# Eight first-layer products, one weight piece and one task's means moved earlier in the lead-in of a fused attention and two-mixture kernel

## The chip, the cores and the metric

The kernel runs on one core of one Trainium2 chip, as one program. The metric is the device time of that program in microseconds (us); the value given for a kernel is the median of its runs.

## What is computed

Three stages follow one another on N = 1536 rows of 512 values (batch 2, sequence 768, 8 heads of 64):

```python
# attention: a band of 15 keys either side, and one summary key per block of 32
k_sum = k.reshape(B, H, nb, block, D).max(axis=3)
v_sum = v.reshape(B, H, nb, block, D).mean(axis=3)
scores_l = scale * (q @ k^T), kept where |i - j| < 16
scores_s = scale * (q @ k_sum^T) + log(32)
x = softmax([scores_l, scores_s]) @ [v, v_sum]
# first mixture, 4 experts, all of them for every row
out += p[:, e:e + 1] * (np.maximum(x @ w1[e], 0.0) @ w2[e])
# second mixture, 8 experts: rows with x @ w_skip > 0 go to the expert of the
# largest logit, the result is added with that expert's probability
```

## The kernel before

**Tasks.** Attention is done in 16 tasks; task a covers one pair of heads and one half (384 rows) of a sequence. Tasks 0 to 3 (`LEAD = 4`) are the four head pairs of the first half, and make the 4 x 128 input columns of the first group of 384 rows of the first mixture. These four are done in the lead-in, before there is any mixture work; tasks 4 to 15 are interleaved with the mixture's first expert.

A task has two halves h (the heads of its pair). On TensorE: `transpose_keys`, `transpose_queries`, `qk(a)` (scores, L1772), `turn(a, h)` (transposes of the probabilities, L1786, after `norm(a, h)`), `pv(a)` (values, L1800). On VectorE: `keys(a)` (the block maxima), `mask(a, h)` (mask and row maximum, L1126), `norm(a, h)` (L1134, L1136, L1138), `low_o(a)` (L1144). On ScalarE: copies of keys and queries, `exps(a, h)` (L864), `evac_t(a, h)` (L870), `high_o(a)` (L875). GpSimd and SyncE issue transfers.

**Two parts for every number.** The mixture's products are made in a fast format. Each operand is split in a high part (rounded to that format) and a low part (the rest), and three products are summed: high by high, high by low, low by high. For the activations, `high_o` and `low_o` make `xt_hi` and `xt_lo`. For w1 of expert 0, GpSimd makes the high part (`high_w1`, a cast, L737) and VectorE the low part (`low_w1`, a subtraction, L1193), piece by piece: piece kc is rows 128 kc to 128 kc + 127 of w1, with all 1024 columns. An F block is 128 of those columns; there are 8. A product of F block f and piece kc is one matrix product of 128 x 128 by 128 x 384.

**Order of work.** It is written by hand for each engine, and semaphores join the engines. GpSimd, on its one queue, copies the block means of the values into the value tiles (`first_sums(a)`, two transfers, L732), loads the pieces of w1 (`first_w1(c)`, L723) and casts them. `first_sums(a)` for a of 2 or 3 waits for `pv(a - 2)`, since it fills the tile which that one read; `pv(a)` waits for it, for the values' windows (`load_windows`, from SyncE), for both `evac_t` of the task, and for `low_o(a - 1)`. `first_w1(1)` waits for the second block of means (`vsum_ok` of 2).

TensorE's lead-in ends with `lead(2)`, that is turn(2,0), qk(3), the queries of task 4, pv(1), turn(2,1), and then

```python
            turn(LEAD - 1, 0)
            pv(LEAD - 2)
            turn(LEAD - 1, 1)
            qk(LEAD)
            pv(LEAD - 1)
```

After that it runs `attend(4, ...)`: the queries of task 5, then `group_steps` for the first group (L1846, L1849, L1852 are F block 0, L1738 to L1740 the others), then turn(4,0), qk(5), turn(4,1). The first two F blocks come before turn(4,0).

VectorE's end of the lead-in is norm(2,1), mask(3,1), norm(3,0), low_o(1), norm(3,1), low_w1 of piece 0, low_o(2), low_w1 of pieces 1 and 2, low_o(3), low_w1 of piece 3, mask(4,0), mask(4,1), norm(4,0). `spare` puts transposes of the identity into some of TensorE's waits (L1889).

Of the kernel before, what the change touches and what calls it, by code (L numbers as in the profile page):

```python
# [15 lines left out]
P = 128  # L16


def sparse_attention_moe_moe(nc, q, k, v, dprobs, w1, w2, w_skip, w_gate, v1, v2, out):
# [102 lines left out]
    with ExitStack() as ctx:  # L122
# [576 lines left out]
        def _(gp):  # L699
# [20 lines left out]
            def first_w1(c):  # L720
                if c:
                    gp.wait_ge(vsum_ok, 2)
                gp.dma_start(early_w1(c), w1[0][c * P:(c + 1) * P, :]).then_inc(first_w1_in[c], 16)  # L723

            def first_sums(a):
                n = task(a)[2]
                gp.wait_ge(vsum_ok, n // 2 + 1)
                if a >= 2:
                    gp.wait_ge(pv_done, a - 1)
                for h in range(2):  # L730
                    row = NB * (2 * (n % 2) + h)
                    gp.dma_start(v_all[a % 2][WK:KW, :, h * DH:(h + 1) * DH],  # L732
                                 v_sum[row:row + NB, n // 2:n // 2 + 1, :].broadcast_to((NB, UH, DH))).then_inc(first_sums_in[a % 2], 16)
# [9 lines left out]
            first_sums(0)  # L743
            first_sums(1)
            first_w1(0)
            first_w1(1)
            first_w1(2)
            first_w1(3)
            high_w1(0)
            first_sums(2)  # L750
            high_w1(1)
            high_w1(2)
            first_sums(3)
# [348 lines left out]
        def _(dve):  # L1102
# [57 lines left out]
            def lead(a):  # L1160
                mask(a + 1, 0)
                norm(a, 1)
                mask(a + 1, 1)
                if a + 2 < LEAD:
                    keys(a + 2)
                norm(a + 1, 0)
                if a:
                    low_o(a - 1)
# [57 lines left out]
            lead(1)  # L1226
            lead(2)
            norm(3, 1)
            low_w1(0, early_w1, [0])
            low_o(2)  # L1230
            low_w1(0, early_w1, [1, 2])
            low_o(3)
# [500 lines left out]
        def _(pe):  # L1733
# [100 lines left out]
            def periods(q):  # L1834

                return [(a, 4 - (a % 2)) for a in range(LEAD + PAIRS * q, LEAD + PAIRS * (q + 1))]

            def group_steps(c, e, b, half, first=False):

                if first and c == 0:  # L1840

                    pe.wait_ge(h_ok, 1)
                    for kc in range(KC):
                        pe.wait_ge(w1_hi_ok, kc + 1)
                        pe.wait_ge(o_hi, kc + 1)
                        mm(ps[:, 0, 0:GT], w1_hi[:, kc, 0:P], xt_hi[:, kc, 0:GT], start=(kc == 0), stop=False)  # L1846
                    for kc in range(KC):
                        pe.wait_ge(o_lo, kc + 1)
                        mm(ps[:, 0, 0:GT], w1_hi[:, kc, 0:P], xt_lo[:, kc, 0:GT], start=False, stop=False)  # L1849
                    for kc in range(KC):  # L1850
                        pe.wait_ge(w1_ok, kc + 1)
                        last = mm(ps[:, 0, 0:GT], w1_lo[:, kc, 0:P], xt_hi[:, kc, 0:GT], start=False, stop=(kc == KC - 1))  # L1852
                    last.then_inc(l1_done, 1)
                    yield
                else:
                    pe.wait_ge(w1_ok, PIECES * e + PIECES)
                for f in range(1 if first and c == 0 else 0, FC):
                    pe.wait_ge(h_ok, FC * c + f + 1)
                    for kc in range(KC):
                        if first and f == 0:  # L1860
                            pe.wait_ge(o_lo, PAIRS * c + kc + 1)
                        cols = (slice(None), bass.ds(PAIRS * b + kc, 1), slice(half * GT, half * GT + GT))
                        w = (slice(None), kc, slice(f * P, (f + 1) * P))
                        last = three(ps[:, f % 2, 0:GT], w1_hi[w], w1_lo[w],
                                     xt_hi[cols].rearrange("p o c -> p (o c)"), xt_lo[cols].rearrange("p o c -> p (o c)"),
                                     kc == 0, kc == KC - 1)
                    last.then_inc(l1_done, 1)
                    yield
                for tt in range(GR):
                    pe.wait_ge(acc_ok, GR * c + tt + 1)  # L1870
                    for f in range(FC):
                        if tt == 0:
                            pe.wait_ge(h_ok, FC * c + f + 3)
                            pe.wait_ge(w2_ok, PIECES * e + f // 2 + 1)
                        rows = (slice(None), f, slice(tt * P, (tt + 1) * P))
                        last = three(ps[:, 2 + (half + tt) % 2, :], h_hi[rows], h_lo[rows], w2_hi[:, f, :], w2_lo[:, f, :], f == 0, f == FC - 1)
                        if f == FC - 1:
                            last.then_inc(l2_done, 1)
                        if f % 4 == 3:
                            yield  # L1880
# [16 lines left out]
            for a in range(LEAD - 1):  # L1897
                spare(a, SPARE[a])
                lead(a)
            turn(LEAD - 1, 0)  # L1900
            pv(LEAD - 2)
            turn(LEAD - 1, 1)
            qk(LEAD)
            pv(LEAD - 1)
            for c in range(G - 1):
                step = group_steps(c, 0, c // HALVES, c % HALVES, True)
# [314 lines left out]
```

## Time and profile before

| | us |
|---|---|
| median of 3 runs | 727.56 |
| runs | 727.91, 727.56, 725.95 |
| the profiled execution, its own time | 727.6 |
| its span | 725.9 |
| TensorE busy in the span | 703.0 (97%) |
| VectorE, ScalarE, GpSimd busy | 403.5, 281.5, 66.2 |

All rows are of the profiled execution, and count from the start of its span, 725.9 us long; the 1.7 us between its time and its span lie outside the span. A row of the timeline gives the start and the length of a run of equal instructions, and in brackets how long the engine had been idle before it and who ended that.

### The profile page before, as it was taken

The numbers are of one execution on the slowest core, as the hardware profiler recorded it, in microseconds if no ns is written. First come the engines' busy times: TensorE is split into PE (matmuls) and PEld (weight loads), VectorE is DVE, ScalarE is ACT, GpSimd is POOL, SyncE is SP. The second block draws the span as 40 slices with busy tenths as digits, with TensorE's granted clock in tenths as the row PEclk, the third lists the DMA queues.
The fourth block names the chain that finished last, engine by engine and source line by source line (L and its number), as shares of the span: only waits on it lengthen the run. The fifth ranks groups of instructions, "written<-read, shape, count | busy, mean of one in ns | idle before, by whom it ended". The sixth has DMA issues, their size and how long they took to land.

```text
span 725.9 us, 12345 instructions
## 1 busy us (share of the span) xinstructions
PE 703.0 (97%) x4499; PEld 580.9 (80%) x4500; DVE 403.5 (56%) x1041; ACT 281.5 (39%) x654; POOL 66.2 (9%) x97
## 2 busy tenths in 40 slices
PE   6599999999999999999999999999999999999997
PEld 5488898898989889988988998899899885444443
DVE  4887584552795684754757364456437317443431
ACT  4745364451345434631621451054036112542430
POOL 2512000000000000000000000100010103233221
PEclk9989999999999999999999999999999999999999
DMA  9985632120708817723977738134630996699900
GB/s 210 213 201 114 135 81 57 39 48 4 287 3 327 333 62 268 295 75 93 427 286 295 261 116 346 63 114 158 247 117 1 361 375 233 242 395 396 375 3 22
DMA packets 92384, 139.36 MB, mean 192 GB/s; under 512 B 55172, under 2 KB 55456, under 8 KB 90656
## 3 DMA queue, kind: packets, MB, share of 16 engines
q1 hardware_dynamic: 89664, 133.89, 53.2%
q0 software_dynamic: 2656, 4.66, 2.0%
q8 instruction: 35, 0.57, 0.3%
q14 instruction: 29, 0.24, 0.1%
HBM read 104.05 MB, written 34.98 MB: 192 GB/s over the span
## 4 chain that ended last, share of the span: by engine, by line
PE 86%; DMA 5%; DVE 3%; issue 2%; SPq 1%; POOL 1%; ACT 1%; POOLq 0%; DVEq 0%
PE ps L1738 15%; PE ps L1740 15%; PE ps L1739 15%; PE ps L1988 8%; PE ps L1990 8%; PE ps L1989 8%; PE ps L2127 4%; PE ps L2099 4%; DMA sets<-in_moe_w 3%; PE ps L1800 2%; PE ps L1772 1%; PE ps L1786 1%; PE ps L1931 1%; DMA v_first<-stage 1%; PE ps L1751 1%
## 5 line engine op out<-in xcount | busy, mean ns | idle before, releaser
L1988 PE MATMUL ps<-xt_hi,wb_hi 128*128 128x384 f32 x336 | 112.7, 336 | 0.0
L1990 PE MATMUL ps<-xt_hi,wb_lo 128*128 128x384 f32 x336 | 112.4, 334 | 0.0
L1989 PE MATMUL ps<-xt_lo,wb_hi 128*128 128x384 f32 x336 | 112.3, 334 | 0.0
L969 ACT ACTIVATE h_raw<-ps 128x384 f32<-128x384 f32 x96 | 47.1, 490 | 116.2 <-PE ps L1990 114.0
L1739 PE MATMUL ps<-v_lo_acc,hb_hi 128*128 128x512 f32 x216 | 84.2, 390 | 0.0
L1365 DVE SCALAR_TENSOR_TENSOR acc<-ps,dp,acc 128x512 f32<-128x512 f32 x36 | 27.0, 750 | 99.3 <-PE ps L1740 99.3
L1350 DVE TENSOR_TENSOR h_raw<-ps,h_raw 128x384 f32<-128x384 f32 x96 | 49.7, 553 | 44.4 <-PE ps L1990 44.3
L975 ACT ACTIVATE hb_hi<-h_raw 128x384 fp32r<-128x384 f32 x96 | 49.0, 525 | 52.5 <-DVE h_raw L1350 52.5
L1988 PEld LDWEIGHTS ps<-xt_hi,wb_hi 128*128 128x128 f32 x336 | 63.1, 188 | 0.4
L1989 PEld LDWEIGHTS ps<-xt_lo,wb_hi 128*128 128x128 f32 x336 | 63.1, 188 | 0.3
L1990 PEld LDWEIGHTS ps<-xt_hi,wb_lo 128*128 128x128 f32 x336 | 63.1, 188 | 0.0
L1355 DVE SCALAR_TENSOR_TENSOR hb_lo<-h_raw,hb_hi 128x384 fp32r<-128x384 f32 x96 | 50.6, 555 | 14.6 <-ACT hb_hi L975 14.4
L1738 PE MATMUL ps<-v_hi_first,hb_hi 128*128 128x512 f32 x144 | 56.8, 395 | 0.0
L1740 PE MATMUL ps<-v_hi_first,hb_lo 128*128 128x512 f32 x144 | 56.1, 390 | 0.0
L2099 PE MATMUL ps<-sets,under 128*64 128x512 f32 x224 | 51.8, 600 | 1.5 <-DVE sets L1679 1.4
L2127 PE MATMUL ps<-sets,acc 128*64 128x256 f32 x448 | 51.6, 382 | 0.7 <-ACT acc L1044 0.7
L783 POOL DMA_INDIRECT route_list<-entry,slot x12 | 12.1, 1008 | 402.2 <-DVE slot L1504 399.4
L1739 PEld LDWEIGHTS ps<-v_lo_acc,hb_hi 128*128 128x128 f32 x216 | 40.6, 188 | 8.2
L2127 PEld LDWEIGHTS ps<-sets,acc 128*64 128x64 f32 x448 | 31.5, 137 | 17.7 <-issue 3.1
L1738 PE MATMUL ps<-xt_hi,w_hi 128*128 128x384 f32 x124 | 43.8, 354 | 0.3 <-DVE h_lo L1202 0.3
L1740 PE MATMUL ps<-v_hi_next,hb_lo 128*128 128x512 f32 x108 | 42.1, 390 | 0.0
L1738 PE MATMUL ps<-v_hi_next,hb_hi 128*128 128x512 f32 x108 | 42.0, 389 | 0.0
(269 smaller groups left out, 1301.0 us busy)
## 6 DMA issues: line engine op xcount, KB each, us to landing
sets<-in_moe_w SPq DMA_DIRECT2D x72, 512.0 KB
w_aside<-wb_hi SPq DMA_DIRECT2D x3, 3584.0 KB, 17.0
w_aside<-wb_lo SPq DMA_DIRECT2D x3, 3584.0 KB, 24.8
wb_hi<-w_aside SPq DMA_DIRECT2D x21, 512.0 KB, 10.8
wb_lo<-w_aside SPq DMA_DIRECT2D x21, 512.0 KB, 11.6
acc<-in_moe_w SPq DMA_DIRECT2D x12, 768.0 KB, 5.3
w_raw<-in_moe_w SPq DMA_DIRECT2D x12, 512.0 KB, 5.4
stage<-in_k SPq DMA_DIRECT2D x16, 192.0 KB, 4.1
```

Source lines behind the costliest of these rows:

```text
L969: nc.scalar.activation(h_raw[:, f, half * GT:(half + 1) * GT], ps[:, bank, 0:GT], ACT.Copy).then_inc(put_by, 1)
L975: nc.scalar.activation(hb_hi[cols], h_raw[cols], ACT.Relu).then_inc(hb_hi_ok, 1)
L1350: TT(to, ps[:, bank, 0:GT], to, ALU.add).then_inc(joined, 1)
L1355: nc.vector.scalar_tensor_tensor(out=hb_lo[cols], in0=h_raw[cols], scalar=0.0, in1=hb_hi[cols].bitcast(F32), op0=ALU.max, op1=ALU.subtract ...
L1738: mm(dst, a_hi, b_hi, start=start, stop=False)
L1739: mm(dst, a_hi, b_lo, start=False, stop=False)
L1740: return mm(dst, a_lo, b_hi, start=False, stop=stop)
L1988: mm(to, wb_hi[w], hi(c), start=(c == 0 and not onto), stop=False, skip_group_check=onto)
L1989: mm(to, wb_hi[w], lo(c), start=False, stop=False, skip_group_check=onto)
L1990: last = mm(to, wb_lo[w], hi(c), start=False, stop=(c == HALF_D - 1), skip_group_check=onto)
L2099: last = mm(ps[j * QT:(j + 1) * QT, 0, 0:FQ], of[:, from_c:from_c + QT], wset[:, 0, at:at + FQ], start=(c == 0), stop=(c == KC - 1))
L2127: last = mm(ps[j * QT:(j + 1) * QT, bank, 0:DQ], ht2[:, at:at + QT], wset[:, 0, to:to + DQ], start=(f == 0), stop=(f == FC - 1))
```

## The change

1. GpSimd: `first_sums(2)` is issued before `first_w1(1)` to `first_w1(3)` and before the first cast, no longer behind them.
2. VectorE: `low_w1` of piece 0 stands in `lead(2)` between mask(3,1) and norm(3,0), no longer behind norm(3,1).
3. TensorE: of the 24 products of F blocks 0 and 1 of the first group, eight are done earlier: piece 0 of both blocks, high and low activations (four products), between turn(2,1) and turn(3,0); piece 1 with the high activations (two) between turn(3,0) and pv(2); piece 1 with the low activations (two) between qk(4) and pv(3). The other 16 stay behind the queries of task 5; both blocks now use their own bank of PSUM at the same time, and the products with the low weights come last. (The words that come with the change speak of ten products; the diff moves eight.)

```diff
@@ GpSimd @@
             first_w1(0)
+            first_sums(2)
             first_w1(1)
             first_w1(2)
             first_w1(3)
             high_w1(0)
-            first_sums(2)
             high_w1(1)
@@ VectorE, lead(a) @@
                 mask(a + 1, 1)
                 if a + 2 < LEAD:
                     keys(a + 2)
+                else:
+                    low_w1(0, early_w1, [0])
                 norm(a + 1, 0)
@@ VectorE @@
             lead(2)
             norm(3, 1)
-            low_w1(0, early_w1, [0])
             low_o(2)
@@ TensorE @@
+            def first_high(f, kc):
+
+                pe.wait_ge(w1_hi_ok, kc + 1)
+                pe.wait_ge(o_hi, kc + 1)
+                mm(ps[:, f, 0:GT], w1_hi[:, kc, f * P:(f + 1) * P], xt_hi[:, kc, 0:GT], start=(kc == 0), stop=False)
+
+            def first_low(f, kc):
+                pe.wait_ge(o_lo, kc + 1)
+                mm(ps[:, f, 0:GT], w1_hi[:, kc, f * P:(f + 1) * P], xt_lo[:, kc, 0:GT], start=False, stop=False)
@@ TensorE, group_steps, first group @@
+                    for f in range(2):
+                        for kc in range(2, KC):
+                            first_high(f, kc)
+                        for kc in range(2, KC):
+                            first_low(f, kc)
+                    for part in (range(KC - 1), range(KC - 1, KC)):
+                        for f in range(2):
+                            for kc in part:
+                                pe.wait_ge(w1_ok, kc + 1)
+                                last = mm(ps[:, f, 0:GT], w1_lo[:, kc, f * P:(f + 1) * P], xt_hi[:, kc, 0:GT], start=False, stop=(kc == KC - 1))
+                            if KC - 1 in part:
+                                last.then_inc(l1_done, 1)
+                    yield
                     yield
                 else:
                     pe.wait_ge(w1_ok, PIECES * e + PIECES)
-                for f in range(1 if first and c == 0 else 0, FC):
+                for f in range(2 if first and c == 0 else 0, FC):
@@ TensorE, end of the lead-in @@
+            pe.wait_ge(h_ok, 2)
+            pe.wait_ge(k_ok, LEAD)
+            for f in range(2):
+                first_high(f, 0)
+                first_low(f, 0)
             turn(LEAD - 1, 0)
+            for f in range(2):
+                first_high(f, 1)
             pv(LEAD - 2)
             turn(LEAD - 1, 1)
             qk(LEAD)
+            for f in range(2):
+                first_low(f, 1)
             pv(LEAD - 1)
```

TensorE at the end of the lead-in, before: turn(2,1), turn(3,0), pv(2), turn(3,1), qk(4), pv(3), queries of task 5, F block 0.

```order
L1786 MATMUL ps<-ident,h_rows 120x128 x3
L1786 MATMUL ps<-ident,stage 120x128 x3
L1800 MATMUL ps<-stage,v_first 64x64 x12
L1786 MATMUL ps<-ident,stage 120x128 x3
L1772 MATMUL ps<-k_high0,stage 64x120 x12
L1800 MATMUL ps<-stage,acc 64x64 x12
L1761 MATMUL ps<-ident,raw_q 128x128 x3
L1846 MATMUL ps<-xt_hi,w1_hi 128x384 x4
```

The same place in the changed kernel, whose line numbers are shifted by one and more (L1843 is `first_high`, L1847 `first_low`).

```order
L1787 MATMUL ps<-ident,h_rows 120x128 x3
L1843 MATMUL ps<-xt_hi,w1_hi 128x384
L1847 MATMUL ps<-xt_lo,w1_hi 128x384
L1843 MATMUL ps<-xt_hi,w1_hi 128x384
L1847 MATMUL ps<-xt_lo,w1_hi 128x384
L1787 MATMUL ps<-ident,stage 120x128 x3
L1843 MATMUL ps<-xt_hi,w1_hi 128x384 x2
L1801 MATMUL ps<-stage,v_first 64x64 x12
L1787 MATMUL ps<-ident,stage 120x128 x3
L1773 MATMUL ps<-k_high0,stage 64x120 x12
L1847 MATMUL ps<-xt_lo,w1_hi 128x384 x2
L1801 MATMUL ps<-stage,acc 64x64 x12
```

Four products stand between the two turns, two ahead of pv(2) and two ahead of pv(3).

GpSimd's queue, the loads and casts of w1 and the copies of the means (`v_first<-stage` is task 2, `acc<-stage` the odd tasks):

```order
 L732 DMA acc<-stage 24x6x64 x2
-L723 DMA acc<-in_moe_w1 128x1024 x4
-L737 CAST w1_hi<-acc 128x1024
+L723 DMA acc<-in_moe_w1 128x1024
 L732 DMA v_first<-stage 24x6x64 x2
-L737 CAST w1_hi<-acc 128x1024 x2
+L723 DMA acc<-in_moe_w1 128x1024 x3
+L737 CAST w1_hi<-acc 128x1024 x3
 L732 DMA acc<-stage 24x6x64 x2
```

The two copies for task 2 now stand behind one load, and three loads and the first cast stand behind them.

VectorE in `lead(2)`, behind the masks of task 3:

```order
 L1126 ISA stage,nmax<-ps,neg_mask 128x120
 L1126 ISA nmax 128x1
+L1195 TENSOR_TENSOR w1_lo<-acc,w1_hi 128x1024
 L1134 TENSOR_SCALAR rsum<-rsum 128x3
 L1136 RECIPROCAL rinv<-rsum 128x3
```

The subtraction of piece 0 stands ahead of norm(3,0).

## Rows read from the trace of the kernel before

**Rows 1.** The page, part 1: busy us, share of the span, instructions.
```profile
PE 703.0 (97%) x4499; PEld 580.9 (80%) x4500; DVE 403.5 (56%) x1041; ACT 281.5 (39%) x654; POOL 66.2 (9%) x97
```

**Rows 2.** Timeline of TensorE, 25 to 49 us: start, us, engine, line, op.
```profile
25.35 0.92 PE L1800 MATMUL ps<-stage,v_first 120*64 120x64 f32 x24 [0.15 <-DMA v_first<-stage]
...
33.20 0.55 PE L1786 MATMUL ps<-ident,h_rows 128*120 128x128 f32 x3 [0.34 <-DVE h_rows L1138]
34.96 0.54 PE L1786 MATMUL ps<-ident,stage 128*120 128x128 f32 x3 [1.21 <-DVE stage L1138]
36.60 1.55 PE L1800 MATMUL ps<-stage,v_first 120*64 120x64 f32 x24 [1.10 <-DMA v_first<-stage]
38.08 0.90 PE L1786 MATMUL ps<-ident,stage 128*120 128x128 f32 x3
38.91 1.48 PE L1772 MATMUL ps<-k_high,stage 64*64 64x120 f32 x24
40.32 1.55 PE L1800 MATMUL ps<-stage,acc 120*64 120x64 f32 x24
...
43.14 0.85 PE L1849 MATMUL ps<-xt_lo,w_hi 128*128 128x384 f32 x4
...
46.64 0.55 PE L1786 MATMUL ps<-ident,h_rows 128*120 128x128 f32 x3
47.12 0.84 PE L1772 MATMUL ps<-k_high,stage 64*64 64x120 f32 x24
48.35 0.54 PE L1786 MATMUL ps<-ident,h_rows 128*120 128x128 f32 x3 [0.38 <-DVE h_rows L1138]
```

**Rows 3.** Busy time by stretch; PEclk is the granted clock, last DMA share and GB/s.
```profile
32.00:36.00 4.00, 1.95 (x31) 1.33 (x30) 3.28 (x18) 3.87 (x16) 2.20 (x4) 0.94 0.81 199
36.00:42.00 6.00, 5.40 (x76) 4.55 (x77) 5.30 (x7) 1.41 (x4) 1.03 (x1) 0.50 0.60 108
42.00:48.00 6.00, 5.96 (x54) 5.37 (x53) 4.56 (x20) 3.91 (x16) 2.45 (x2) 0.97 0.98 277
```

**Rows 4.** The chain of work that ended last, 25 to 37 us: start, us, what.
```profile
26.10 1.14 POOL acc L723 x3
...
27.77 1.04 POOL w_hi L737
...
29.41 6.95 DMA v_first<-stage
```

**Rows 5.** Transfers issued at 26.0 to 26.6 and 34.2 to 35.3 us: KB, us to landing.
```profile
acc<-in_moe_w POOLq DMA_DIRECT2D x1, 512.0 KB, 4.5
...
acc<-stage POOLq DMA_DIRECT2D x2, 36.0 KB, 2.6
```

**Rows 6.** Timeline of GpSimd, 32 to 38 us.
```profile
33.06 1.04 POOL L737 CAST w_hi<-acc 128x1024 fp32r<-128x1024 f32 x1 [1.40 <-DMA acc<-in_moe_w]
34.05 1.20 POOL L732 DMA_DIRECT2D acc<-stage  x2
35.98 1.05 POOL L737 CAST w_hi<-acc 128x1024 fp32r<-128x1024 f32 x1 [0.73 <-DMA acc<-in_moe_w]
```

**Rows 7.** Timeline of VectorE, 29 to 44 us.
```profile
29.63 0.53 DVE L1138 TENSOR_TENSOR h_rows<-h_rows,rinv 128x360 f32<-128x360 f32 x1
...
33.70 0.42 DVE L1134 TENSOR_SCALAR rsum<-rsum 128x3 f32<-128x3 f32 x1
...
34.82 0.55 DVE L1144 TENSOR_TENSOR xt_lo<-ps,xt_hi 128x384 fp32r<-128x384 f32 x1
35.96 0.17 DVE L1134 TENSOR_SCALAR rsum<-rsum 128x3 f32<-128x3 f32 x1 [0.59 <-ACT stage L864]
...
36.38 1.04 DVE L1138 TENSOR_TENSOR stage<-stage,rinv 128x360 f32<-128x360 f32 x1
...
39.19 2.35 DVE L1193 TENSOR_TENSOR w_lo<-acc,w_hi 128x1024 fp32r<-128x1024 f32 x2
...
42.91 1.22 DVE L1193 TENSOR_TENSOR w_lo<-acc,w_hi 128x1024 fp32r<-128x1024 f32 x1
```

More of the change, by code:

```diff
@@ L1836, in periods @@
                 return [(a, 4 - (a % 2)) for a in range(LEAD + PAIRS * q, LEAD + PAIRS * (q + 1))]
+            def first_high(f, kc):
[5 more added lines that the diff above has]
+                mm(ps[:, f, 0:GT], w1_hi[:, kc, f * P:(f + 1) * P], xt_lo[:, kc, 0:GT], start=False, stop=False)
             def group_steps(c, e, b, half, first=False):
                 if first and c == 0:
[L1842 to L1853, printed above, removed]
+                    for f in range(2):
[11 more added lines that the diff above has]
+                    yield
                     yield
```

## The prediction

> **What bounds the kernel now.** I read the page's shares first: TensorE is busy for 97% of the span [rows 1]. Time can therefore be won only where TensorE waits or runs slowly, and the edit touches one such place, the last 15 us of the lead-in. The timeline of TensorE there [rows 2] is the view that counts. Names: turn(a,h), qk(a), pv(a) are the transposes, scores and value products of task a. TensorE ends turn(2,1) at 33.75 and waits 1.21 us for VectorE's norm(3,0); it does turn(3,0) at 34.96 and waits 1.10 us for a transfer; pv(2) starts at 36.60. From there it has no wait until turn(4,1), which is 0.38 us late at 48.35. Behind 48.35 it meets nothing in the next microseconds that this edit moves, so my measure is the start of turn(4,1): what it gains or loses there, the span gains or loses.
>
> The second thing is the clock [rows 3]. It was granted in full over nearly all of 32 to 36, at 0.50 (the 1.2 GHz level) from 36 to 42, and in full again after it. The fall came after the two waits with one short turn between them. Its price stands in rows 2: pv takes 1.55 us low and 0.92 full (25.35), a turn 0.90 and 0.55, qk 1.48 and 0.84.
>
> The third is why pv(2) waited. The chain [rows 4] goes through GpSimd: three weight loads issued from 26.10, the cast of piece 0, and only then the two copies of the means for task 2. The second was issued at 29.41 and took 6.95 us behind the weights. The same queue's copies for task 3, issued from 34.05 on when most of the weights had landed, took 2.6 us [rows 5].
>
> **The change part by part.**
>
> *The means sent sooner (first_sums(2) ahead of first_w1(1)).* They need pv(0), which ends at 26.27 (25.35 and 0.92 in rows 2), so GpSimd issues them at about 26.5 to 27.8. Nothing but the tail of other traffic is ahead of them; by the rows for the same size (2.6 us best, 6.95 worst) the last lands between 29.8 and 34.1, in either case before 36.4. The 1.10 us wait on the transfer goes. What is pushed back by these two issues and the wait for pv(0) is 1.7 us: the loads of pieces 1 to 3 start at 27.8 instead of 26.10 [rows 4], and as the first of them took 4.5 us [rows 5] and the casts of rows 6 each began when their piece was there, I put the cast of piece 1 at 32.3 and those of pieces 2 and 3 at 34.8 and 37.7 for 33.06 and 35.98. The cast of piece 0 goes from 27.77 to about 29.5 or 30.0.
>
> *The low weight piece moved up (low_w1 of piece 0 between mask(3,1) and norm(3,0)).* VectorE has no room there: norm(3,0) began at 33.70, straight behind the masks, and it is what turn(3,0) waits for. Piece 0 costs 1.17 us (two took 2.35, rows 7), so turn(3,0) goes from 34.96 to 36.1. low_o(1) stands behind it (34.82, done at 35.37) and pv(2) needs that as well, so the pv(2) that the transfer releases is held by VectorE instead: what replaces the transfer's wait is mostly this. The piece's old place, behind norm(3,1), was free to move: its 1.17 us there go to low_w1 of pieces 1 and 2, which nothing on this path waits for.
>
> *Casts against norms.* VectorE and GpSimd hold each other up: the multiplication of norm(3,1) took 1.04 us while the cast of 35.98 ran, 0.53 elsewhere, and the short L1134 took 0.42 us at 33.70 under the cast of 33.06 and 0.17 at 35.96, just ahead of one [rows 6, 7]. The masks, which read the scores from PSUM, lose nothing. The casts now fall elsewhere: that of piece 0 on norm(2,0)'s multiplication (29.63 to 30.16, rows 7), that of piece 1 on norm(2,1)'s, that of piece 2 on low_w1 or norm(3,0). Each meeting costs 0 to 0.9 us according to who is first; on the path up to turn(3,0) the ends are 0 and 1.6. (The upper one: the cast of piece 0 from 29.45 to 30.5 sends norm(2,0) back by 0.74; that of piece 1 from 32.3 then catches L1134 of norm(2,1), 0.3; that of piece 2 catches low_w1 or norm(3,0), some 0.6.) I take 0.65, nearer to what single meetings showed (0.25 and 0.51). So turn(3,0) is at 36.75.
>
> The Trainium skill has a rule that speaks against this change, in "GPSIMD Engine Reference", Specifications: GpSimd's SBUF interfaces are shared with VectorE, and VectorE instructions with two SBUF inputs contend for them. low_w1 has two such inputs, so by that rule the piece that was moved up may itself be stopped by a cast or stop one; no row shows that yet, only the norms. Taken at its word at every cast it would make the sum the upper end, turn(3,0) at 37.7, rival 2 below.
>
> *The products.* Eight are moved: after turn(2,1) four (two F blocks, high and low, piece 0), after turn(3,0) two, after qk(4) two. At full clock a product takes 0.17 us of TensorE (four last 0.85, each overlapping the next and 0.33 long by itself, so three steps of 0.17). The four take 0.7 us inside a wait that is now 2.3 us or more, and cost nothing. If the wait were gone they would cost 0.7. The two behind turn(3,0) take 0.35, under low_o(1), which ends 0.41 after turn(3,0)'s start: nothing, or 0.1. The two behind qk(4) are on the path: 0.35. The 16 left after the queries, for 24 before, free 1.4 us of TensorE, and I cost that at nothing: turn(4,0) needs norm(4,0), whose masks stand on VectorE behind low_o(3) and low_w1 of piece 3 (42.91), and that chain ends at 46.6, where TensorE arrives now. TensorE will wait there instead.
>
> *The clock.* The wait before turn(3,0) grows, but four products stand in it, and the one before pv(2) shrinks. I take it that the grant stays full.
>
> *The sum.* turn(3,0) 36.75; low_o(1) done 37.2; pv(2) 37.2 to 38.1 (0.92); norm(3,1), which takes 0.95 without a meeting (norm(3,0) took 1.2 with its 0.25), also done 38.1; turn(3,1) 38.1; qk(4) 38.6; two products from 39.35; pv(3) could start at 39.7. Its means are issued behind the cast of piece 2, at about 36.2 and 36.8, and land 2.6 later, 39.4, or later behind piece 3; for that and for a meeting of norm(3,1) with the last cast I add 0.3: pv(3) at 40.0 for 40.32. From pv(3) to turn(4,1) the chain took 8.03 us (40.32 to 48.35) with pv(3) at 1.55; at 0.92 it is 7.4. So turn(4,1) starts at 47.4 for 48.35: 0.95 us won. The profiled execution took 727.6 us (span 725.9), and the median of the three runs is 727.56, so the two agree: **726.6 us**, and 725.9 to 727.3 with this case's own bounds (0.7 us of meetings and landings either way). A measurement of this kernel tells about 0.3%, 2.2 us, from no change, so this is no change.
>
> **The rivals.**
> 1. *No meetings, means on time.* turn(3,0) 36.1, pv(2) 36.55, turn(3,1) 37.5, pv(3) 39.0, turn(4,1) 46.4: 1.95 us won, 725.6. For it: casts wait for data, and their times could fall under the masks. Against: three casts and five pieces of two-input work lie in 7 us.
> 2. *All meetings, or the means of task 3 late.* turn(3,0) at 37.7, pv(3) at 41.1, turn(4,1) at 48.5: 727.7, the gain wholly given back. The late transfer alone does it too: it would have to land at 41.0, 4.2 us after its issue, between the 2.6 and 6.95 of the rows.
> 3. *Slower: the clock falls all the same.* The place is the wait before turn(3,0), which low_w1 lengthens. If the grant is 0.50 from about 36.7 on, pv(2) runs 37.2 to 38.75, turn(3,1) to 39.6, qk(4) to 41.0, two products (0.33 each) to 41.65, and pv(3) at 1.55 puts turn(4,1) at 49.7: 1.3 us lost, 728.9. For it: before, the grant fell behind a shorter wait. Against: four products fill a third of it. It decides when the clock row behind turn(3,0) reads 0.50.
> 4. *It does not do what it says.* If TensorE's order before pv(2) had no bearing, because a later wait absorbs it all, the time is 727.6. Rows 2 show no such wait in front of 48.35 but the one of 0.38; a later one would have to be new.
>
> **How the numbers follow.** Forecast 0.50, rival 1 0.17, rival 2 0.14, rival 3 0.14, rival 4 0.05. The runs shown lie 2 us apart (725.95 to 727.91), so a median may itself be off by half a microsecond. The range reaches from rival 1 less 0.4, 725.2, to rival 3, 728.9. Faster by over 0.3% (below 725.4) needs rival 1 and luck: 0.10. Slower by over 0.3% (above 729.8) needs rival 3 with late means or meetings: 0.05. The rest, 0.85, is within.
>
> **What would show it.** Right: TensorE's timeline has four products right behind turn(2,1); turn(3,0) starts 1 us or more later than 34.96 and its releaser is VectorE; pv(2) has no wait on a transfer; the windows of 36 to 42 read 1.00; TensorE waits about 1 us before turn(4,0), released by VectorE; turn(4,1) starts near 47.4. L1138 over 0.6 us before 36 would show a meeting. Wrong: turn(3,0) at its old time, a clock of 0.50 behind it, pv(3) released by a transfer, or a turn(4,1) that moved while the span did not.

## The result and the profile after

| | us |
|---|---|
| kernel before, median of 10 runs | 726.40 (725.03 to 728.22) |
| changed kernel, median of 10 runs | 729.36 (728.36 to 731.30) |
| ratio | 1.0040, 95% interval 1.0028 to 1.0053 |
| profiled execution of the changed kernel | 728.39, span 726.7 |

The change costs 0.4%, 3 us. The forecast was 726.6 and no change, with a range up to 728.9: the sign was wrong and the time lies above the range.

TensorE's share is as before; its busy time is 1.7 us more. The page of the changed kernel, part 1, answers to [rows 1]:

```profile
PE 704.7 (97%) x4499; PEld 581.3 (80%) x4500; DVE 406.4 (56%) x1041; ACT 281.3 (39%) x654; POOL 66.4 (9%) x97
```

The timeline of TensorE in the changed kernel, to be laid beside [rows 2] (L1787 is a turn, L1773 qk, L1801 pv, L1843 and L1847 the moved products):

```profile
33.11 0.54 PE L1787 MATMUL ps<-ident,h_rows 128*120 128x128 f32 x3 [0.34 <-DVE h_rows L1138]
...
34.01 0.34 PE L1847 MATMUL ps<-xt_lo,w_hi 128*128 128x384 f32 x1
36.79 0.54 PE L1787 MATMUL ps<-ident,stage 128*120 128x128 f32 x3 [2.44 <-DVE stage L1138]
37.09 0.60 PE L1843 MATMUL ps<-xt_hi,w_hi 128*128 128x384 f32 x2
37.62 1.17 PE L1801 MATMUL ps<-stage,v_first 120*64 120x64 f32 x24
39.09 0.89 PE L1787 MATMUL ps<-ident,stage 128*120 128x128 f32 x3 [0.30 <-DVE stage L1138]
39.92 1.48 PE L1773 MATMUL ps<-k_high,stage 64*64 64x120 f32 x24
41.33 1.01 PE L1847 MATMUL ps<-xt_lo,w_hi 128*128 128x384 f32 x2
42.26 1.55 PE L1801 MATMUL ps<-stage,acc 120*64 120x64 f32 x24
...
49.13 0.55 PE L1787 MATMUL ps<-ident,h_rows 128*120 128x128 f32 x3 [1.52 <-DVE h_rows L1138]
...
50.64 0.54 PE L1787 MATMUL ps<-ident,h_rows 128*120 128x128 f32 x3 [0.19 <-DVE h_rows L1138]
...
53.40 0.92 PE L1801 MATMUL ps<-stage,v_first 120*64 120x64 f32 x24
```

and pv(4) in the kernel before:

```profile
51.12 0.92 PE L1800 MATMUL ps<-stage,v_first 120*64 120x64 f32 x24
```

turn(3,0) starts at 36.79 for 34.96, pv(2) at 37.62 for 36.60 and without a wait on a transfer, pv(3) at 42.26 for 40.32, turn(4,0) at 49.13 behind a wait of 1.52 us, and turn(4,1) at 50.64 for 48.35: 2.29 us later; pv(4) behind it is 2.28 us later. From there the two executions run in parallel. The two answers by line give the first and last start of TensorE's products of the later experts (L1988 before, L2009 after), and they are 2.3 us apart at both ends:

```profile
L1988 PE MATMUL ps<-xt_hi,wb_hi x336: 332/334/423, 213.8 to 561.4; 128*128 128x384 f32 x168
```

```profile
L2009 PE MATMUL ps<-xt_hi,wb_hi x336: 332/334/423, 216.1 to 563.7; 128*128 128x384 f32 x168
```

The second mixture starts 2.3 us later as well (602.3 and 604.6), and its length is what varies from one execution to the next. From there to the end of the span it took 123.6 us in this execution of before, and between 122.0 and 123.1 in the thirteen other profiled executions of this document (span less that start). So the profiled spans, 725.9 and 726.7, differ by only 0.8 us although the lead-in lost 2.3. The start of pv(4) is the better measure: what was lost or won by then was still there at the second mixture. The table at the end of the experiments gives it, with that of turn(4,1).

VectorE in the changed kernel, beside [rows 7]:

```profile
33.57 1.46 DVE L1195 TENSOR_TENSOR w_lo<-acc,w_hi 128x1024 fp32r<-128x1024 f32 x1
34.96 1.00 DVE L1134 TENSOR_SCALAR rsum<-rsum 128x3 f32<-128x3 f32 x1
...
37.12 1.14 DVE L1134 TENSOR_SCALAR rsum<-rsum 128x3 f32<-128x3 f32 x1
...
44.86 1.76 DVE L1195 TENSOR_TENSOR w_lo<-acc,w_hi 128x1024 fp32r<-128x1024 f32 x1
```

GpSimd in the changed kernel, beside [rows 6] (L723 loads of w1, L732 copies of means, L737 casts of w1, L741 casts of w2):

```profile
27.84 1.23 POOL L732 DMA_DIRECT2D v_first<-stage  x2 [5.44 <-PE ps L1801]
29.06 1.68 POOL L723 DMA_DIRECT2D acc<-in_moe_w  x3
30.78 1.04 POOL L737 CAST w_hi<-acc 128x1024 fp32r<-128x1024 f32 x1
32.92 1.04 POOL L737 CAST w_hi<-acc 128x1024 fp32r<-128x1024 f32 x1 [1.10 <-DMA acc<-in_moe_w]
34.17 1.77 POOL L737 CAST w_hi<-acc 128x1024 fp32r<-128x1024 f32 x1 [0.21 <-DMA acc<-in_moe_w]
35.88 1.29 POOL L732 DMA_DIRECT2D acc<-stage  x2
37.17 1.05 POOL L737 CAST w_hi<-acc 128x1024 fp32r<-128x1024 f32 x1
44.51 1.04 POOL L741 CAST w_hi<-acc 128x1024 fp32r<-128x1024 f32 x1 [6.28 <-DMA acc<-in_moe_w]
```

An L1134 works on three columns and takes 0.15 to 0.17 us when nothing is in its way. Read the two lists together, in order of time. low_w1 runs into the cast of 32.92 and takes 1.46 instead of 1.2. The cast of 34.17 is held by it and lasts 1.77 instead of 1.04. norm(3,0)'s L1134 is held by that cast for 0.83 us. norm(3,1)'s, at 37.12, is held by the cast of 37.17 for 0.97. The piece of 44.86 is held by the cast of 44.51 for 0.5.

The clock fell here too, at 38.1 us where it had fallen at 35.5 before [rows 3], and was at 0.50 for as long (6.8 us):

```profile
32.00:36.00 4.00, 2.02 (x31) 1.00 1.01 324
36.00:42.00 6.00, 4.91 (x58) 0.68 0.57 94
42.00:48.00 6.00, 5.61 (x45) 0.76 0.98 250
```

(Columns: the stretch, its length, TensorE busy, granted clock, share of the transfer engines, GB/s.)

### The profile page after: what moved, and what is told of

It is laid out like the page before. It is cut to its first block, busy times and chain, and to the rows that moved or that the text cites. A ratio compares the mean times of both kernels' runs of the same rounds, so it can differ in the third digit from the quotient of the medians.

```text
span 726.7 us, 12350 instructions
## 1 busy us (share of the span) xinstructions
PE 704.7 (97%) x4499; PEld 581.3 (80%) x4500; DVE 406.4 (56%) x1041; ACT 281.3 (39%) x654; POOL 66.4 (9%) x97
## 4 chain that ended last, share of the span: by engine, by line
PE 92%; DVE 5%; ACT 1%; issue 1%; DMA 0%; POOL 0%; SPq 0%; POOLq 0%; DVEq 0%
PE ps L1739 15%; PE ps L1741 15%; PE ps L1740 15%; PE ps L2009 8%; PE ps L2011 8%; PE ps L2010 8%; PE ps L2148 7%; PE ps L2120 7%; PE ps L1801 2%; PE ps L1773 2%; PE ps L1787 1%; PE ps L1952 1%; PE ps L2133 1%; PE ps L1752 1%; DVE acc L1156 1%
## 5 line engine op out<-in xcount | busy, mean ns | idle before, releaser
L2009 PE MATMUL ps<-xt_hi,wb_hi 128*128 128x384 f32 x336 | 112.7, 336 | 0.0
L2009 PEld LDWEIGHTS ps<-xt_hi,wb_hi 128*128 128x128 f32 x336 | 63.1, 188 | 0.4
```

Of the source, the lines that this page charges most:

```text
L2009: mm(to, wb_hi[w], hi(c), start=(c == 0 and not onto), stop=False, skip_group_check=onto)
```

## The experiments

Twelve runs in three groups (one of them is the changed kernel once more), each compared with the kernel before on the same chip. Theory A: the loss comes from VectorE, where low_w1 of piece 0 and GpSimd's casts stand on the path of norm(3,0) and norm(3,1). Theory B: it comes from GpSimd's order alone, which makes loads, casts and the means of task 3 late. Theory C: the clock. The ratio of two medians can differ from the ratio given by up to 0.06%.

### First group: parts of the change

**The means alone (sums_only).**

```diff
             first_w1(0)
+            first_sums(2)
             first_w1(1)
...
             high_w1(0)
-            first_sums(2)
             high_w1(1)
```

> The kernel before with one edit: the two copies of the means for task 2 are issued ahead of the loads of w1 pieces 1 to 3. Theory A (the loss comes from VectorE: low_w1 of piece 0 ahead of norm(3,0), made longer by GpSimd's casts, and the clock falls in that wait): without low_w1 there, turn(3,0) stays near 35.0, pv(2) follows at 35.6 instead of 36.6 and turn(4,1) starts about 1 us earlier than 48.35 if the clock still falls, 2 to 3 us if not; total 0.5 to 1.5 us below the kernel before. Theory B (the loss comes from GpSimd's order: the loads of w1 now wait for pv(0), so casts and the means of task 3 are late): turn(4,1) at 49 or later and the total 1 us or more above the kernel before. Theory C (the clock's phase alone): the same total within 0.5 us.

Measured: ratio 1.0009 (0.9993 to 1.0025). turn(3,0) at 35.57 with an L1134 of 0.89 us under a cast of 33.68, pv(2) at 36.13 without a transfer's wait. Then the transfer's wait came back one task later:

```profile
40.54 1.55 PE L1800 MATMUL ps<-stage,acc 120*64 120x64 f32 x24 [1.17 <-DMA acc<-stage]
```

pv(3) waits for the means of task 3, which GpSimd issued at 36.37 instead of 34.05. That is no gain of 1 us, so not A as put; a loss of 1 us, as B had it, lies inside the interval. The 1.10 us wait before pv(2) was exchanged for one of 1.17 before pv(3).

**low_w1 alone (low_only).**

```diff
                 if a + 2 < LEAD:
                     keys(a + 2)
+                else:
+                    low_w1(0, early_w1, [0])
                 norm(a + 1, 0)
...
             norm(3, 1)
-            low_w1(0, early_w1, [0])
             low_o(2)
```

> The kernel before with one edit: low_w1 of piece 0 stands on VectorE ahead of norm(3,0) instead of behind norm(3,1). Theory A: turn(3,0) at 36.1 to 36.8, pv(2) at 36.7 to 37.3 since the transfer of 36.4 is late anyway, the wait before turn(3,0) about 2.5 us with nothing in it, clock at 0.50 behind it; turn(4,1) 0.3 to 1.3 us later than 48.35 and the total 0.3 to 1.5 us above the kernel before. Theory B: no change in GpSimd's order, so the same total within 0.3 us. Theory C: within 0.5 us.

Measured: 1.0016 (1.0001 to 1.0030), as theory A had it; the interval reaches down to the 0.3 us that B allowed. low_w1 took 2.34 us instead of 1.2, norm(2,1) had already met a cast (L1134 0.97 us), and turn(3,0) started at 38.18, 1.4 us later than A expected. turn(4,1) was only 1.2 us later than in the execution of before, which had lost 1.10 us to the transfer and had its clock low for 6.8 us against 3.4 here.

**The products alone (products_only).** TensorE's part of the diff and nothing else.

> The kernel before with one edit: the eight products stand at their new places on TensorE; GpSimd's and VectorE's orders are those of before. If the products cost nothing and do not hold the clock up: turn(3,0) 35.0, pv(2) 36.6, turn(4,1) within 0.5 us of 48.35 (the two products ahead of pv(3) cost 0.35 at the full clock, 0.7 at half), total within 0.7 us above. If they hold the clock at full: turn(4,1) 1.5 to 2 us earlier, total 1 to 2 us below the kernel before.

Measured: 0.9979 (0.9964 to 0.9993); the medians are 725.83 and 726.98. The products are the good part of the change. The profiled execution does not show how: its time, 727.13, is among the longest of the twelve, turn(4,1) started at 48.84 for 48.35, and the clock was low for 3.4 us instead of 6.8. What all twelve runs show of the clock stands under spares_only.

**Without low_w1 (no_low_move).** The changed kernel with VectorE's order of before.

> The changed kernel with low_w1 of piece 0 put back behind norm(3,1); the means are sent sooner and the eight products stand at their new places. Theory A: turn(3,0) near 35.0, pv(2) at 35.6 to 35.9, clock kept or fallen later, turn(4,1) 1 to 3 us earlier than 48.35; total 0.5 to 2.5 us below the kernel before, 3 to 5 below the changed one. Theory B: total still 1 us or more above the kernel before.

Measured: 1.0011 (0.9993 to 1.0030). The clock stayed full from 30 us on in the profiled execution, and turn(4,1) still started at 49.19 for 48.35. So theory A is too narrow: taking low_w1 back recovers 0.3% of the 0.4%, but not the gain that A expected nor the one that the products give by themselves. In VectorE's timeline of this kernel the same meetings stand at norm(3,0) and norm(3,1), without any weight piece ahead of them:

```profile
33.99 0.59 DVE L1134 TENSOR_SCALAR rsum<-rsum 128x3 f32<-128x3 f32 x1
...
34.82 1.36 DVE L1138 TENSOR_TENSOR stage<-stage,rinv 128x360 f32<-128x360 f32 x1
...
36.58 1.54 DVE L1134 TENSOR_SCALAR rsum<-rsum 128x3 f32<-128x3 f32 x1
```

### Second group: the casts taken out of the way

**Without the sooner means (no_sums_move).** The changed kernel with GpSimd's order of before.

> The changed kernel with GpSimd's old order: low_w1 of piece 0 ahead of norm(3,0) and the eight products stay moved. The single edits measured +0.1% (means), +0.2% (low_w1) and -0.2% (products), and the whole change +0.4%. If the three simply add, this one is within 0.1% of the kernel before. If the loss needs both the later casts and the piece ahead of norm(3,0) (a meeting on VectorE's path, theory A), it is 0.3 to 0.5% below the changed kernel. If low_w1 alone undoes the products' gain, it is +0.1 to +0.3% against the kernel before.

Measured: 1.0018 (1.0006 to 1.0030), the last of the three cases. GpSimd's new order costs 0.2%, on top of low_w1; the three single edits (+0.1, +0.2, -0.2%) do not add up to the +0.4% of the whole.

**The changed kernel again (after_again).** Nothing edited.

> The changed kernel itself, on the same chip as the three beside it. Both theories: +0.25 to +0.5% against the kernel before, turn(3,0) at 36 to 38 and the clock at 0.50 behind it.

Measured: 1.0039 (1.0024 to 1.0054). The clock stayed full until 49 us in this execution:

```profile
36.00:42.00 6.00, 4.30 (x82) 1.00 0.50 89
42.00:48.00 6.00, 4.91 (x52) 1.00 0.95 249
```

and turn(4,1) still started at 49.24, 0.89 us later than before. Then the clock fell, at 49.2:

```profile
48.00:54.00 6.00, 5.01 (x49) 0.72 1.04 265
```

```profile
49.24 0.90 PE L1787 MATMUL ps<-ident,h_rows 128*120 128x128 f32 x3 [0.99 <-DVE h_rows L1138]
...
53.35 0.92 PE L1801 MATMUL ps<-stage,v_first 120*64 120x64 f32 x24
```

From turn(4,1) to pv(4) took 4.11 us here and 2.76 in the first execution, so 1.35 of the 2.2 us by which pv(4) is late are the clock's. That turn(4,1) was late with a full clock is the work of the meetings, which were longer here:

```profile
34.73 1.00 DVE L1134 TENSOR_SCALAR rsum<-rsum 128x3 f32<-128x3 f32 x1
...
35.98 1.10 DVE L1138 TENSOR_TENSOR stage<-stage,rinv 128x360 f32<-128x360 f32 x1
...
37.87 1.51 DVE L1138 TENSOR_TENSOR stage<-stage,rinv 128x360 f32<-128x360 f32 x1
...
47.43 0.97 DVE L1134 TENSOR_SCALAR rsum<-rsum 128x3 f32<-128x3 f32 x1 [0.56 <-ACT h_rows L864]
```

So the clock is not what makes turn(4,1) late. That it is not the cause of the 0.4% either is told better by all runs than by one: each run lists its mean granted clock, and the median of that figure is 0.995 for the kernel before on each chip, 0.9945 for the changed kernel and 0.995 here.

**Two casts on ScalarE (casts_scalar).** The changed kernel, with the casts of w1 pieces 2 and 3 moved to ScalarE's idle time.

```diff
 GpSimd
-            high_w1(2)
             first_sums(3)
-            high_w1(3)
 ScalarE
+            def high_w1(c):
+                act.wait_ge(first_w1_in[c], 16)
+                act.wait_ge(w1_hi_ok, c)
+                nc.scalar.activation(w1_hi[:, c, :], early_w1(c), ACT.Copy).then_inc(w1_hi_ok, 1)
...
             exps(LEAD - 1, 1)
+            high_w1(2)
             high_o(LEAD - 2)
             evac_t(LEAD - 1, 0)
             evac_t(LEAD - 1, 1)
+            high_w1(3)
```

> The changed kernel with the casts of w1 pieces 2 and 3 done by ScalarE, in its idle time behind the exponentials of task 3 and behind its last evacuation, instead of by GpSimd. GpSimd then casts only pieces 0 and 1. If meetings of GpSimd's casts with VectorE make turn(3,0) late (theory A): L1134 of norm(3,0) and of norm(3,1) take 0.2 instead of 1.0 and 1.1 us, turn(3,0) starts at 35.8 to 36.2 instead of 36.8, and the total is 1 to 2 us below the changed kernel. If VectorE's two-input work only waits for its operands, nothing moves: within 0.5 us of the changed kernel.

Measured: 1.0001 (0.9988 to 1.0013), 2.9 us below the changed kernel beside it (726.57 and 729.46), more than the 1 to 2 us expected. This is the experiment that decides. Everything of the change is still there, and two instructions stand on another engine. VectorE's timeline of this kernel (L1139 is its L1134, L1200 its low_w1):

```profile
33.87 1.59 DVE L1200 TENSOR_TENSOR w_lo<-acc,w_hi 128x1024 fp32r<-128x1024 f32 x1
35.38 0.23 DVE L1139 TENSOR_SCALAR rsum<-rsum 128x3 f32<-128x3 f32 x1
...
36.77 0.16 DVE L1139 TENSOR_SCALAR rsum<-rsum 128x3 f32<-128x3 f32 x1
```

The two short instructions take 0.23 and 0.16 us for 1.00 and 1.14. turn(3,0) at 36.44 came out only a little earlier, since low_w1 is still ahead of it and met the cast of piece 1; norm(3,1) no longer held turn(3,1) up, and turn(4,1) started at 48.55 for 50.64.

Two other things moved with the casts. GpSimd issued the means of task 3 at 34.33 instead of 35.88; but pv(3) had not waited for them in either execution of the changed kernel, so that is not the gain. And the clock was low for 3.4 us instead of 6.8; the median over the runs is 0.997 instead of 0.995, which by the estimate under spares_only is worth about 0.6 of the 2.9 us.

**Means by SyncE, casts by ScalarE, products moved (prod_sp_casts).** The kernel before with the eight products, `first_sums(2)` and `first_sums(3)` issued by SyncE just ahead of `load_windows(2)` and `load_windows(3)`, and the two casts on ScalarE.

> The kernel before with the eight products moved, the copies of the means of tasks 2 and 3 issued by SyncE ahead of the windows of the same task instead of by GpSimd behind the weights, and the casts of pieces 2 and 3 on ScalarE. The weights are loaded at 26.1 as before, and VectorE's order is that of before. Theory A: no cast and no issue on GpSimd next to norm(3,0) and norm(3,1), so turn(3,0) at 35.0, pv(2) at 35.8 without a wait on a transfer, turn(4,1) 1 us or more earlier than 48.35; total 1.5 to 3 us below the kernel before, and below the kernel with the products alone. If meetings do not matter: no better than the products alone (0.2% below the kernel before).

Measured: 0.9986 (0.9974 to 0.9999). turn(3,0) at 34.94, pv(2) at 35.77, turn(4,1) at 47.02, all as expected. The total was not: it gained 1.3 us of the 1.5 to 3, and is not below the products alone (0.9979). TensorE's timeline shows where the next wait stood:

```profile
51.00 0.92 PE L1814 MATMUL ps<-stage,v_first 120*64 120x64 f32 x24 [1.32 <-DMA v_first<-stage]
```

### Third group: what the clock and the casts are worth by themselves

**The casts alone (casts_only).** The kernel before with the two casts on ScalarE.

> The kernel before with one edit: the casts of w1 pieces 2 and 3 are done by ScalarE instead of GpSimd. If GpSimd's casts also cost the kernel before something: norm(3,0) and norm(3,1) without long instructions, 0.25 and 0.5 us less on VectorE; the transfer of the means of task 2 still ends the wait for pv(2), so the total gains at most 0.3 us: within 0.1% of the kernel before. If moving the casts were a gain by itself, whatever the order, the 0.4% that it gave the changed kernel should appear here too.

Measured: 0.9985 (0.9972 to 0.9999), a little more than the 0.1% allowed. The kernel before had meetings too. Moving the two casts is worth 0.15% to it and 0.4% to the changed kernel.

The expectation failed in one more point: pv(2) started at 35.43, right behind turn(3,0), and did not wait for its transfer, although the means were issued at 28.92, no sooner than before (28.75). Their landing in this execution, and in the one of before (median of the two copies, us):

```profile
v_first<-stage POOLq DMA_DIRECT2D x2, 36.0 KB, 5.5
```

```profile
v_first<-stage POOLq DMA_DIRECT2D x2, 36.0 KB, 6.5
```

In all five executions beside that of before with this order of GpSimd's queue (casts_only, spares_only, products_only, low_only, no_sums_move) it was 5.4 to 5.8, and in none of them did pv(2) wait for it. Only casts_only is a direct test, since in the others pv(2) came at 36.28 or later for other reasons; for those the landing speaks. The second copy was issued at 29.5 to 29.9, so it landed at 35.1 to 35.8 (an estimate, issue plus landing), where it was 36.4 in the execution of before, and turn(3,0) ended at 35.5 there. So most of the wait of 1.10 us that the change takes away was that of one execution.

**Transposes instead of products (spares_only).**

```diff
+            pe.wait_ge(q_copied, LEAD + 1)
+            for _ in range(7):
+                nc.tensor.transpose(ps[:, 2, PS:PS + P], ident[:, :], ident[:, :])
             turn(LEAD - 1, 0)
+            for _ in range(4):
+                nc.tensor.transpose(ps[:, 2, PS:PS + P], ident[:, :], ident[:, :])
             pv(LEAD - 2)
```

> The kernel before with eleven transposes of the identity that nobody reads in TensorE's two waits, seven ahead of turn(3,0) and four ahead of pv(2), where the kernel with the moved products alone has six of its eight products. No work is moved. If the 0.2% of the moved products comes from keeping the clock up or shortening the stretch at 0.50, this gives 0.1 to 0.3% too. If it comes from TensorE having less to do in front of turn(4,0), this gives nothing or costs up to 0.1%.

Measured: 0.9985 (0.9971 to 0.9999). Eleven useless transposes give as much as eight useful products, within the intervals. The granted clock of this execution, TensorE alone:

```profile
32.00:36.00 4.00, 3.00 (x43) 1.00 0.59 164
36.00:42.00 6.00, 5.23 (x90) 1.00 0.71 143
```

It was 0.50 in the second stretch before [rows 3]. Over all runs the median of the mean granted clock is 0.998 here and 0.998 with the products alone, for 0.995 in the kernel before. Among the runs of the kernel before, 0.001 more of it goes with about 0.3 us less (a line through each chip's runs gives 0.29, 0.34 and 0.31, one run at 0.945 left out), so 0.003 is worth about 0.9 us: an estimate, from a correlation, and about the whole gain of the transposes (medians 725.90 and 726.75) and most of that of the products (1.15 us). So the gain of the products is consistent with the clock alone, and that they take work off TensorE was not needed for it, as the prediction had said of the 16 left.

**Means by SyncE, all casts on GpSimd (prod_sp).**

> The kernel before with the eight products moved and the copies of the means of tasks 2 and 3 issued by SyncE; GpSimd keeps all four casts of w1. Against the same kernel with the casts of pieces 2 and 3 on ScalarE (0.14% below the kernel before) it tells what the casts cost where VectorE has no weight piece ahead of norm(3,0). Meetings matter: turn(3,0) after 35.3, a long L1134 or L1138 in it, and a total up to 1 us above that kernel. They don't: the same.

Measured: 0.9991 (0.9978 to 1.0003). turn(3,0) at 35.80, 0.9 us later than with the casts on ScalarE (34.94), behind a multiplication of norm(3,0) that took 1.04 us, but pv(3) 0.3 us earlier and turn(4,1) at 46.76. The totals of the two cannot be told apart. In this order, with no weight piece ahead of norm(3,0) and no issue on GpSimd beside the casts, the meeting is not seen in the total.

**SyncE's queue reordered as well (best2).** `load_windows(4)` and `load_sums(4)` ahead of `first_w2(0)` and `first_w2(1)`.

> As the kernel with the products moved, the means issued by SyncE and two casts on ScalarE, and in addition SyncE issues the windows and the means of task 4 ahead of the first two pieces of w2. In the kernel without this last edit turn(4,1) started at 47.0 instead of 48.35, but pv(4) then waited 1.32 us for the means of task 4 (51.0). If that wait is where the gain was given back: pv(4) at 49.7 to 50.0 without a wait, total 1 us lower, 724.6, 2 us below the kernel before. If the next transfer in line (w2, or task 5's) takes its place: a wait of about 1 us later, the total as without the edit.

Measured: 0.9988 (0.9979 to 0.9997), 725.70. The wait for the means of task 4 was gone: pv(4) started at 49.31 for 51.00. Of these 1.7 us a new wait of TensorE on VectorE's low part of h took 0.54, and 1.1 were still there at the start of the second mixture (601.2 for 602.3); but the median did not follow (725.70, forecast 724.6), and why stays open. No version is clearly better than the products alone (0.9979), and those already beat both kernels.

The starts that matter, one profiled execution each, with the stretch of the lead-in at 0.50 between 30 and 60 us, and the median over all runs of the mean granted clock:

| kernel | turn(3,0) | pv(3) | turn(4,1) | pv(4) | at 0.50, us | clock, all runs | ratio |
|---|---|---|---|---|---|---|---|
| before | 34.96 | 40.32 | 48.35 | 51.12 | 6.8 | 0.995 | 1 |
| changed | 36.79 | 42.26 | 50.64 | 53.40 | 6.8 | 0.9945 | 1.0040 |
| changed, again | 37.14 | 41.23 | 49.24 | 53.35 | 3.4 (from 49) | 0.995 | 1.0039 |
| no_sums_move | 37.99 | 42.98 | 50.57 | 53.34 | 3.4 | 0.995 | 1.0018 |
| no_low_move | 36.24 | 40.75 | 49.19 | 51.96 | 0 | 0.9965 | 1.0011 |
| low_only | 38.18 | 42.22 | 49.57 | 52.51 | 3.4 | 0.995 | 1.0016 |
| sums_only | 35.57 | 40.54 | 48.90 | 51.67 | 6.8 | 0.9945 | 1.0009 |
| casts_scalar | 36.44 | 41.34 | 48.55 | 52.05 | 3.4 | 0.997 | 1.0001 |
| products_only | 36.31 | 41.27 | 48.84 | 51.60 | 3.4 | 0.998 | 0.9979 |
| casts_only | 34.87 | 39.25 | 47.09 | 49.84 | 3.4 | 0.997 | 0.9985 |
| spares_only | 35.37 | 39.27 | 47.03 | 49.84 | 0 | 0.998 | 0.9985 |
| prod_sp | 35.80 | 39.26 | 46.76 | 49.48 | 0 | 0.998 | 0.9991 |
| prod_sp_casts | 34.94 | 39.58 | 47.02 | 51.00 | 0 | 0.998 | 0.9986 |
| best2 | 34.84 | 38.90 | 46.54 | 49.31 | 0 | 0.999 | 0.9988 |

The clock of all runs also counts a fall of 3.4 us or more near 20 us, where TensorE's program is the same in every kernel and which 8 of the 14 profiled executions have, and the last microseconds. One execution is not a median: the clock falls at another moment in each, and no_sums_move, whose profiled execution looks like that of the changed kernel, is 0.2% faster over its runs. The ratios decide, the starts explain.

## Why the prediction was wrong

**The frame held.** Between 60 us and the second mixture TensorE waited once, for 0.3 us and in every kernel alike, and what the lead-in lost or won by pv(4) was still there at the second mixture (in best2 less the wait of 0.54).

**The means (a step that failed: the gain was not there).** "The 1.10 us wait on the transfer goes" took one execution for the kernel. It did go, but in five other executions with the old order, told of under casts_only, the copies landed about a microsecond sooner, so sending the means sooner bought nothing as a rule (sums_only: 1.0009), and it delayed everything behind it. The issue came at 27.84 instead of the 26.5 assumed: GpSimd issued 0.6 us after pv(0) had ended, and pv(0) itself ran later in that execution (26.29), where the clock was at 0.50 from 21.0 to 24.5. In the second execution it came at 27.18. The loads of w1 so came 2.3 to 3.0 us later, not 1.7.

**low_w1 (right).** turn(3,0) was forecast at 36.75 and came at 36.79 and 37.14, released by VectorE.

**The meetings (the step that failed).** The text took "0.65, nearer to what single meetings showed" up to turn(3,0), and 0.3 for everything behind. Up to turn(3,0) the result was near: 0.7 and 1.0 us above the 36.1 without meetings. The meetings themselves were longer (0.26 on low_w1 and 0.83 on L1134, with none at norm(2,0) and norm(2,1)); but the 34.96 that the forecast started from held one of 0.25 already, which it counted twice. Behind turn(3,0) the step was mis-sized. The meeting of norm(3,1) with the cast of piece 3 held it for 0.97 us, where 0.3 was allowed together with late means, and the last weight piece met a cast of w2 for 0.5, where nothing was. In the second execution norm(3,1) was held for 0.98 and norm(4,1) for 0.8. The mistake has a form: in the profiled execution of before the meeting of norm(3,1) was hidden, because pv(2) was late on its transfer and turn(3,1) stood behind pv(2). With the transfer on time norm(3,1) decides when turn(3,1) starts. I had removed the cover and not charged what it hid. TensorE's own work had slipped too, though, and its wait there was only 0.30 and 0.56 us. Rival 2 named this mechanism but gave it 727.7, too little, and 0.14.

**The products (small).** I put the two behind turn(3,0) at "nothing, or 0.1". From the start of turn(3,0) to that of pv(2) took 0.83 us with them and 0.56 in the kernel with the casts alone moved, so 0.27; norm(3,1) ended later still, so this was not on the path. The two ahead of pv(3), put at 0.35, took 0.54 at the full clock (40.69 to 41.23 in the second execution). That the 16 remaining would buy nothing was right: TensorE waited 1.52 us ahead of turn(4,0), forecast "about 1".

**The clock (wrong in the profiled execution).** "I take it that the grant stays full" failed in one of two executions up to 49 us, and there pv(3) started 1.0 us later than in the other; in the other it fell at 49.2. Rival 3 gave 728.9 for this, the nearest of all the numbers, but the clock does not explain the 0.4%: over all runs its median is that of the kernel before (0.9945 and 0.995 for 0.995), and moving two casts removed the loss while the clock still fell.

**The sum.** Forecast 47.4 for turn(4,1), measured 50.64 and 49.24. In the second execution, with a full clock up to there, the 1.8 us are the meetings: 0.4 more than allowed up to turn(3,0), 0.98 at norm(3,1), 0.8 at norm(4,1), less the 0.3 allowed; the products add 0.2, and 0.2 go the other way. In the first, the 3.2 us are 1.2 of meetings (0.97 and 0.5, less the 0.3 allowed), 0.2 of the products and about 2.0 of the clock (1.4 from turn(3,1) to pv(3), where the second execution took 1.79 us and this one 3.17, and 0.6 in pv(3) itself), with 0.2 the other way. The forecast was helped by luck besides: it started from three runs with a median of 727.56, where the ten runs of that kernel have 726.40. The change was forecast at -0.95 us and measured at +3.0, so the miss is 3.9 us, and the high start hid 1.2 of it.

**Why the whole is worse than the parts.** What the runs show is that the whole loss needs the casts on GpSimd. With them there it is 0.39%, without the two later ones 0.01%. The same move gives the kernel before 0.15%, and nothing that can be told apart where the means are issued by SyncE (prod_sp and prod_sp_casts). So what the casts cost depends on the order around them, and is largest in this one, where later loads bring casts onto norm(3,0) and norm(3,1), whose waits no transfer covers any more. One more part of the difference can be read from the clock: the products are worth -0.2% by themselves with a clock of 0.998, and in the changed kernel the clock is that of the kernel before, so the longer waits appear to have taken that gain back. That is argued, not tested alone. The same holds for the 0.15% that is left between the changed kernel and the kernel before when both have the two casts on ScalarE (1.0001 against 0.9985): that it is the 1.2 us of low_w1 on VectorE's path is argued from the difference. For the meetings the rule of the Trainium skill ("GPSIMD Engine Reference", Specifications) was the right one to follow: the trace agrees, with 2.43 us for a low_w1 in no_sums_move where 1.2 is normal. L1134, which has a single tensor input, was held for up to 1.4 us too; the same row also names VectorE's 2-port performance mode, and no run here shows whether L1134 runs in it.

## What to carry to other kernels

A wait on a transfer in one profiled execution is a guess until a second execution shows it; here the transfer landed about a microsecond sooner in five of six. Before taking a wait away, list what ran under it and what it cost. When work moves on GpSimd's queue, look at the long casts behind it and at which VectorE instructions they will then meet, and try the cast on ScalarE if that has a gap. Put a filler into the waits of TensorE alone first: it may hold all of the gain. Compare the granted clock over all runs, not only in the profiled one.

## What the runs showed that was not expected

A VectorE instruction can be held longer than a cast lasts. In the kernel with the products alone, L1138 took 2.02 us for 0.53; it started in the middle of GpSimd's issue of two copies and ended after the cast that followed. VectorE's row and GpSimd's two:

```profile
34.24 2.02 DVE L1138 TENSOR_TENSOR stage<-stage,rinv 128x360 f32<-128x360 f32 x1
```

```profile
33.61 1.20 POOL L732 DMA_DIRECT2D acc<-stage  x2 [1.21 <-PE ps L1800]
34.81 1.05 POOL L737 CAST w_hi<-acc 128x1024 fp32r<-128x1024 f32 x1
```

The same pattern, an instruction that begins in the second half of such an issue with a cast right behind it, stands in low_only (2.34 us), no_sums_move (2.43), no_low_move (1.54) and both executions of the changed kernel (1.14 and 1.51). Where no cast followed at once, as at 29.63 in the kernel before [rows 7], the issue held nothing up. In sums_only it went the other way once: a weight piece at 37.14 was not held, and the cast of 37.65 lasted 1.61 us instead. What decides who goes first stays open.
